# Moving the two arrays of split weights by 64 bytes in SBUF, in a kernel of attention, a dense feed-forward and routed experts

## The reference

```python
# attention: 4 batches, 8 heads, 576 positions, 64 dims; half the heads see the last 32 positions,
# half see every 32nd position
scores = scale * q @ k.T;  scores = where(mask, scores, -1e9);  attn = softmax(scores)
x = (attn @ v)                                  # laid out as (2304, 512)
# dense feed-forward, 512 -> 2048 -> 512
h = x @ w_in;  g = h * (1 / (1 + exp(-1.702 * h)));  x = g @ w_out
# routed experts: 8 experts, 512 -> 1024 -> 512, one expert for each token that is computed
do_compute = x @ w_skip > 0;  xc = x[do_compute];  logits = xc @ w_gate
e_idx = argmax(logits);  gate_w = softmax(logits)[e_idx]
h = relu(xc[mask] @ w1[e]);  y[mask] = gate_w[mask] * (h @ w2[e]);  out[do_compute] = xc + y
...
```

## The kernel before

| array | first byte | modulo 128 | role |
|---|---|---|---|
| `w_hi`, `w_lo` | 16512, 82048 | 0, 0 | split weights |
| `w_raw` | 147584 | 0 | raw weights, slots 0 to 3 |
| `more_raw` | 171584 | 64 | raw weights, slots 4 to 7 |
| `ident` | 155776 | 0 | moving operand of the transposes |
| `x_hi`, `x_lo` (both buffers) | 194368 and on | 64 | moving in `up` |
| `gated`, `g_hi`, `g_lo` | 210752 and on | 64 | stationary in `down` |
| `xe_hi`, `xe_lo`, `h_hi`, `h_lo`, `relu_h`, `xg` | 163392 and on | 64 | expert stage |

## Time and profile before

### The profile page before, as it was taken

One profiled execution on the slowest core, in us unless ns is written; L12 is line 12 of the kernel. 1 busy time (PEld: TensorE's weight loads), 2 busy tenths in 40 slices (PEclk: granted clock), 3 DMA queues, 4 the chain that ended last, 5 costly groups with the idle time before them and its releaser, 6 DMA issues.

```text
span 717.1 us, 14298 instructions
## 1 busy us (share of the span) xinstructions
PE 671.2 (94%) x4533; PEld 576.4 (80%) x4534; DVE 392.6 (55%) x1363; ACT 369.4 (52%) x1043; POOL 159.3 (22%) x211
## 2 busy tenths in 40 slices
PE   3889999999999999999999999999978899999990
PEld 3678888888888889889898988998857688887870
DVE  4867764555456434253343433445575876577664
ACT  4778766555656333333333333344436865457661
POOL 5345312231223002010010000100222433303431
PEclk9999999999999999999999999999999999999996
DMA  7547634223321331102001020023118886557761
GB/s 254 190 131 251 208 121 162 73 73 132 102 73 40 119 121 30 60 1 89 1 19 70 0 88 0 0 74 89 46 46 260 281 259 212 188 179 240 243 210 40
DMA packets 48215, 85.60 MB, mean 119 GB/s; under 512 B 7618, under 2 KB 11714, under 8 KB 48160
## 3 DMA queue, kind: packets, MB, share of 16 engines
q1 hardware_dynamic: 43664, 79.20, 33.6%
q0 software_dynamic: 3952, 4.65, 2.2%
q10 hardware_dynamic: 544, 1.05, 0.4%
HBM read 70.84 MB, written 18.52 MB: 125 GB/s over the span
## 4 chain that ended last, share of the span: by engine, by line
PE 81%; issue 5%; DVE 4%; POOL 4%; ACT 2%; DMA 2%; POOLq 1%; DVEq 0%; SPq 0%; ACTq 0%
PE ph L1345 27%; PE px L1358 27%; PE pe_h L1445 8%; PE py L1471 7%; PE pscore L1295 3%; PE ptrans L1304 2%; PE pctx L1317 2%; DMA w_raw<-we 1%; PE ph L1369 1%; PE phT L1457 1%; POOL probs L651 1%; DMA xg<-x_dram,gather_slots 1%; DVE w_lo L952 1%; ACT w_hi L772 1%; PE pxT L1425 1%
## 5 line engine op out<-in xcount | busy, mean ns | idle before, releaser
L1345 PE MATMUL ph<-x_hi,w_hi 128*128 128x256 f32 x576 | 166.2, 289 | 0.8 <-DVE x_lo L1013 0.8
L1108 DVE SCALAR_TENSOR_TENSOR gated<-gated,ph 128x256 f32<-128x256 f32 x144 | 60.5, 420 | 188.1 <-ACT gated L849 188.0
L1345 PE MATMUL ph<-x_lo,w_hi 128*128 128x256 f32 x576 | 160.6, 279 | 0.0
L1345 PE MATMUL ph<-x_hi,w_lo 128*128 128x256 f32 x576 | 160.4, 279 | 0.0
L1358 PE MATMUL px<-w_hi,g_hi 128*128 128x512 f32 x288 | 117.7, 409 | 0.0
L1345 PEld LDWEIGHTS ph<-x_hi,w_hi 128*128 128x128 f32 x576 | 108.5, 188 | 7.9 <-issue 3.3
L1358 PE MATMUL px<-w_hi,g_lo 128*128 128x512 f32 x288 | 113.6, 394 | 0.0
L1358 PE MATMUL px<-w_lo,g_hi 128*128 128x512 f32 x288 | 113.0, 392 | 0.0
L1345 PEld LDWEIGHTS ph<-x_lo,w_hi 128*128 128x128 f32 x576 | 108.9, 189 | 3.6
L1345 PEld LDWEIGHTS ph<-x_hi,w_lo 128*128 128x128 f32 x576 | 108.8, 189 | 0.0
L849 ACT ACTIVATE gated<-ph 128x256 f32<-128x256 f32 x144 | 54.9, 381 | 102.3 <-PE ph L1345 102.3
(11 more groups left out here) (201 smaller groups left out, 1101.9 us busy)
## 6 DMA issues: line engine op xcount, KB each, us to landing
w_raw<-we SPq DMA_DIRECT2D x72, 256.0 KB, 3.2
more_raw<-we SPq DMA_DIRECT2D x72, 256.0 KB, 4.0
w_raw<-wf SPq DMA_DIRECT2D x32, 256.0 KB, 3.9
vs<-vw SPq DMA_DIRECT2D x16, 384.0 KB, 3.4
qs<-qT SPq DMA_DIRECT2D x16, 288.0 KB, 3.8
ks<-kT SPq DMA_DIRECT2D x16, 288.0 KB, 4.2
xT_dram<-x_stage SPq DMA_DIRECT2D x16, 288.0 KB, 3.1
x_lo<-xT_dram SPq DMA_DIRECT2D x8, 512.0 KB, 3.8
```

The source lines that it names most:

```text
L1108: nc.vector.scalar_tensor_tensor(gated[s % 2][:, :], gated[s % 2][:, :], 1.0, ph[s % 2][:, 0:TT], ALU.add, ALU.mult).then_inc(gated_done, 1)
L1345: last = nc.tensor.matmul(ph[f % 2][:, 0:TT], up_w(w, k, f), x[p][:, k, :], start=(at == 0 and n == 0), stop=(at == KD - 1 and n == 2))
```

## The change

Sixteen floats of padding are put ahead of the two arrays and sixteen behind them. `w_hi` and `w_lo` thereby begin 64 bytes later, at 64 modulo 128. `w_raw` and all that follows begin 128 bytes later, so they keep their remainder modulo 128. No instruction is added, removed or moved; only the addresses in them differ, and nothing reads or writes the padding.

```diff
+        sb("gap_before_weights", [P, 16])
         w_hi = sb("w_hi", [P, NCH * CH], F32R)
         w_lo = sb("w_lo", [P, NCH * CH], F32R)
+        sb("gap_behind_weights", [P, 16])
         w_raw = sb("w_raw", [P, RAW, CH])
```

## The result

The changed kernel takes 725.8 us (median of 4 runs, 724.31 to 727.74) where the one before takes 717.65: ratio 1.0115, 95% interval 1.0091 to 1.0139. It is slower by 1.15%, outside of the range that was forecast and on the side of the rival with 0.22. The profiled execution took 724.31 us with a span of 722.7, 5.6 us more than the profiled one of before, and is the fastest of the four; the other 2.5 us between the medians lie in executions without a profile, where no trace tells their place.

A forecast was written before the change was run, and what follows sets the result against it. The prediction took TensorE's matmuls, 81% of what ended last, to bound the kernel. All terms were taken as 0, so it forecast no change, a median of 717.6 us, with a range of 713.6 to 724.5 us.

The forecast's parts named there:

- the rival with 0.22: Rival: moving stream and weight load beginning in one half of 128 bytes collide; 721.6 or 727.6 us, chance 0.22.
- item 3, the pair: TensorE's moving stream and weight load both beginning at 64 modulo 128, in 3216 matmuls; cost taken as 0.
- the colliding pair: Rival of chance 0.22: TensorE's two reads collide; 4.0 us from `up`, 10 us with 512 columns too, 727.6 us.
- The other rival: TensorE's two streams disturb each other today, not when beginning alike; 714.0 us, or 711.1 with `up`; chance 0.16.
- item 1: TensorE's moving stream at another place, 1488 matmuls: likelier 0, at most 2.4 ns each, 3.6 us gained.
- Items 4 to 6: ScalarE's copy to `w_hi`, VectorE's `w_lo`, DMA landings: each taken as 0; bounds 0.06 us for VectorE, 1.6 us for DMA.

The follow-up runs named there:

- e3: Kernel before with the weights in place and all that follows them moved by 128 bytes; 725.55 us, ratio 1.0094.
- f1: Kernel before with the weights in place and all that follows them moved by 256 bytes; 718.39 us, ratio 1.0001.
- g1: Kernel before with the token arrays moved by 64 bytes and all behind them by 256; 725.75 us, ratio 1.0083.
- f3: Changed kernel with the token arrays moved by 192 bytes more, `up` distance 192 again; 719.89 us, ratio 1.0024.
- f4: Kernel before with `g_hi`, `g_lo` and the expert arrays moved by 64 bytes, `down` and experts at distance 0; 719.92 us, ratio 1.001.
- g2: Kernel before with only the expert arrays from `xe` on moved by 64 bytes, experts at distance 0; 717.6 us, ratio 0.9979.

## Why the prediction was wrong

**What bounds the kernel** was read rightly: 3216 matmuls on the changed arrays with no cover, and a mean of 0.7 ns on each as the point from which it decides. It came to 1.7 ns a matmul or more (5.6 us of span / 3216).

**The step that failed is item 3, the pair.** It named the right spot and took 0 for it, on an argument of rates: the moving stream goes through both halves of 128 bytes twice while the load goes through them once, so that the start should not matter. The argument had two faults. It took over the modulus 128 from the words of the change; e3 and f1 show that 128 bytes matter and 256 do not. And it averaged over the phase of two streams that it had itself seen to start in step; with a fixed phase the same meeting would recur in every matmul, and nothing would average out. (That the meeting of the two reads is what costs is the likely reading; no run shows it directly.) It said so under the rivals, as what speaks for a collision, and gave it too little weight. In its place the runs show a cost: with the distance of `up` alone moved to 0, and weights, `g` and experts as before, `up` goes to 120 ns and a tile to 47.44 us (g1), and the change loses 6.2 us in the dense stage.

**The list of moved distances was short by one.** The change does not only bring the weights nearer to all else by 64 bytes. What lies behind them moves by 128, so tokens less weights went from 192 to 0 modulo 256.

**The size.** The bound of the colliding pair took the slower level in the trace, 117.3 ns, for the worst: 4.0 us from `up`. The changed kernel has 120 through nearly the whole group. By the medians of an ordinary step `up` takes 47 ns more and `down` 13, and 57 ns is what a tile shows per step; the dense stage as a whole loses 6.2 us. The prediction looked for such a cost in the first matmuls of each group. It is in the last seven of `up`, 113 to 120 ns; the first five together take what they took. For 512 columns the bound had 4 ns on each of 1488 matmuls, 6.0 us. `down` pays 2 ns, and the experts pay nothing: they run at 227 to 229 ns instead of 229. In `down` the 13 ns do not come from its own distance alone, since with the same distance of 0 and `up` at 192 (f3, f4) it runs at 227 to 229. That the measured 725.8 us lies near this rival's 727.6 is luck, since the sum behind it is made of other parts.

**The other rival** (the streams disturb each other today) has its small truth in the experts: distance 0 is better than 64 by 2 ns in the median and 0.6 ns in the mean (g2), a quarter of the 2.4 ns of item 1. Its sign of being right, a tile of 46.3 us or less, came in no run.

**Items 4 to 6** held: ScalarE at 614 at least, VectorE at 682, landings of 3.2 and 3.9 us (3.2 and 4.0 before). The Trainium skill, in SBUF — State Buffer, section "Who interferes with whom", calls TensorE's two read ports independent. The runs disagree as far as its pitch goes: g1, which differs from the kernel before in the tokens' distance to their neighbours alone, is slower by 0.83%. The Trainium skill, in DMA: Bandwidth & Descriptors, section "How a descriptor splits into AXI transactions", would have `w_raw` land sooner, if its rule holds for writes; the median stays at 3.2 us. That settles little: with `w_raw` at its old place modulo 256 other traces have 3.1 to 3.4 us, a scatter as large as the 6% that was estimated.

**What stays open.** Why 192 is good for 256 columns and 0 for 512, and why `up` needs 64 in `down` for its quick level. That the load beside the stream is the partner follows from which arrays were moved against which, not from a run in which the loads are missing; none was made.

## What to carry to other kernels

Where TensorE is the bound, an array's place is part of its cost, and so is padding or a new small tensor anywhere ahead of it: it shifts all that is allocated later. Compare the start of the moving operand with that of the stationary one modulo 256, here for fp32r, keep that distance fixed while other edits are measured, and try a few others for each kind of matmul; the pitch in one trace tells them apart, where the total needs many runs: one stretch at half clock took 1.65 us in the profile after, more than the smallest of these effects. Take the distance from one piece to its next return in the chain rather than the duration of a single piece; a median of 2 ns was 0.6 ns in the mean.

## What was not expected of the hardware

Equal fp32r matmuls of 256 columns ran at 113 to 120 ns, and of 512 columns with the experts at 227, 229 or 233 ns (medians), at the full clock, in kernels that differ only in where their arrays begin. The distance of the two operands modulo 256 orders them. Of eight distances tried for `up`, one (192) has the quick level, 46.6 us a tile, and the seven others lie within 47.1 to 47.6 us. Even at 192 the level depends on the matmuls before: with `down` at distance 0 instead of 64, `up` runs at 117 to 118 instead of 113 ns.
